# Turning the q and k tiles of an attention and mixture-of-experts kernel as F32R instead of F32 operands

## What is computed

```python
def _attn_ref(q, k, v, centroids):            # q, k, v: (2, 8, 768, 64); centroids: (8, 16, 64)
    q_assign = argmax(einsum('bhsd,hcd->bhsc', normed(q), normed(centroids)), axis=-1)
    k_assign = argmax(einsum('bhsd,hcd->bhsc', normed(k), normed(centroids)), axis=-1)
    mask = q_assign[:, :, :, None] == k_assign[:, :, None, :]
    scores = where(mask, q @ k.T / 8, -1e9)
    return softmax(scores) @ v

x = attention output, as 1536 tokens of 512
idx = argmax(normed(x) @ normed(expert_emb).T / tau)      # one of 8 experts for each token
x = gate * (relu(x @ w1[idx]) @ w2[idx])                  # w1: 512 to 1024, w2: 1024 to 512
out = ((x @ w_a) * (x @ w_b)) @ w_out                     # 512 to 1536 and back
```

## Time and profile before

| | us |
|---|---|
| median of three executions | 971.63 |
| lowest, highest | 966.73, 979.37 |
| the profiled execution | 973.64 |
| span of its instructions | 971.8 |
| mean granted TensorE clock, of full speed | 0.939 |

### The profile page before, as it was taken

The page is one execution under the profiler, slowest core; times in us unless marked ns, Lnnn a source line. Parts: engine busy times, 40 slices in busy tenths (PEclk is TensorE's granted clock), DMA queues, the critical chain, the costliest instruction groups (busy, mean ns, idle before and its releaser), DMA issues.

```text
span 971.8 us, 11830 instructions
## 1 busy us (share of the span) xinstructions
PE 880.1 (91%) x4205; PEld 620.6 (64%) x4206; DVE 513.0 (53%) x683; ACT 293.4 (30%) x558; POOL 225.8 (23%) x175
## 2 busy tenths in 40 slices
PE   5799989999899989509999999969999999999998
PEld 2455555555445554207777777757888888888886
DVE  4667888777888755626566665534321311131111
ACT  3133333333333334503434444423121211121111
POOL 6045655655665442150000000020000100000000
PEclk9579999988999989858999999988999999999999
DMA  4122222222221121366555555652000200010001
GB/s 123 50 70 67 71 68 75 73 78 72 75 67 48 48 82 60 140 222 237 199 199 204 202 196 206 211 183 74 0 1 1 87 1 1 0 44 1 1 1 43
DMA packets 41105, 86.93 MB, mean 89 GB/s; under 512 B 4216, under 2 KB 10584, under 8 KB 41056
## 3 DMA queue, kind: packets, MB, share of 16 engines
q1 hardware_dynamic: 39136, 79.99, 25.4%
q0 software_dynamic: 1920, 6.29, 1.9%
HBM read 60.53 MB, written 17.83 MB: 81 GB/s over the span
## 4 chain that ended last, share of the span: by engine, by line
PE 80%; DVE 11%; issue 6%; DMA 1%; ACT 0%; SPq 0%; DVEq 0%; POOL 0%; ACTq 0%
PE bank L1414 7%; PE bank L1415 7%; PE bank L1416 7%; PE bank L1214 4%; PE pair L1161 4%; PE bank L1354 3%; PE first_pair L1345 3%; PE first_pair L1346 3%; PE first_pair L1347 3%; PE bank L1355 3%; PE bank L1356 3%; PE first_pair L1199 3%; PE first_pair L1201 3%; DVE has_tmp L890 2%; PE bank L1131 2%
## 5 line engine op out<-in xcount | busy, mean ns | idle before, releaser
L1088 DVE TENSOR_TENSOR g_sb<-bank,a_sb 128x512 f32<-128x512 f32 x36 | 24.9, 692 | 196.7 <-PE bank L1416 196.7
L1414 PE MATMUL bank<-x_hi,wt 128*128 128x512 f32 x288 | 115.0, 399 | 1.4 <-DVE x_lo L1057 1.4
L1415 PE MATMUL bank<-x_lo,wt 128*128 128x512 f32 x288 | 114.6, 398 | 0.0
L1416 PE MATMUL bank<-x_hi,wt 128*128 128x512 f32 x288 | 114.5, 398 | 0.0
L844 DVE TENSOR_REDUCE neg_max<-pair 128x1 f32<-128x768 f32 x93 | 88.5, 951 | 45.8 <-PE pair L1161 45.7
L346 POOL TENSOR_TENSOR prob_sum<-prob_sum,prob 128x768 f32<-128x768 f32 x56 | 102.5, 1831 | 11.6 <-ACT prob L582 9.6
L959 DVE TENSOR_TENSOR wt<-w_raw,wt 128x2048 fp32r<-128x2048 f32 x41 | 92.9, 2287 | 10.2 <-ACT wt L661 9.8
L582 ACT ACTIVATE prob<-first_pair 128x384 f32<-128x384 f32 x128 | 59.6, 486 | 83.7 <-PE first_pair L1201 56.6
L1214 PE MATMUL bank<-prob,v_sb 128*64 128x384 f32 x384 | 83.8, 520 | 0.0
L1161 PE MATMUL pair<-kc,qb 96*128 96x384 f32 x186 | 61.7, 417 | 6.1 <-DVE neg_max L844 5.2
L1414 PEld LDWEIGHTS bank<-x_hi,wt 128*128 128x128 f32 x288 | 54.6, 190 | 15.1 <-DVE x_lo L1057 1.8
(11 more groups left out here) (212 smaller groups left out, 1666.1 us busy)
## 6 DMA issues: line engine op xcount, KB each, us to landing
w_raw<-in_moe_w_dram SPq DMA_DIRECT2D x32, 1024.0 KB, 5.2
x_slots<-zeros SPq DMA_DIRECT2D x10, 512.0 KB, 3.7
x_slot<-x_slots SPq DMA_DIRECT2D x18, 256.0 KB, 4.0
y_slots<-y_sb SPq DMA_DIRECT2D x16, 256.0 KB, 4.5
q_raw<-in_q_dram SPq DMA_DIRECT2D x16, 192.0 KB, 2.4
k_raw<-in_k_dram SPq DMA_DIRECT2D x16, 192.0 KB, 2.5
v_sb<-in_v_dram SPq DMA_DIRECT2D x16, 192.0 KB, 2.3
qb<-qa SPq DMA_DIRECT2D x16, 192.0 KB, 2.6
```

The lines of the kernel that those rows point to most:

```text
L1414: pe.matmul(to[:, :], w[0], x2_hi[:, kk, :], start=(kk == 0), stop=False)
L1415: pe.matmul(to[:, :], w[0], x2_lo[:, kk, :], start=False, stop=False)
L1416: last = pe.matmul(to[:, :], w[1], x2_hi[:, kk, :], start=False, stop=(kk == KD - 1))
```

## The change

A second identity, `ident_r`, is declared as F32R. DVE writes it in the setup with one more copy (128 by 128), placed between L786 and L787, and raises a new semaphore `setup_ident`. PE waits for that at the head of its program, behind its wait for `setup_in`. The transposes of L1131 take the tile as F32R, as it is declared, with `ident_r` as moving operand, and write through an F32R view of the bank; ACT and DVE read the bank as F32 as before. Pool's two subtractions (L496, L500) write to the F32R tile without the view as F32, so their results are rounded to F32R. The other transposes keep F32 and `ident`.

```diff
+        ident_r = sb("ident_r", [P, P], F32R)
...
+        setup_ident = sem("setup_ident")
...
             def low_parts(n):
...
-                pool.tensor_tensor(q_split[s][:, :, D:2 * D].bitcast(F32),
+                pool.tensor_tensor(q_split[s][:, :, D:2 * D],
                                    q_raw[s][:].rearrange("p (t d) -> p t d", t=NT),
                                    q_split[s][:, :, 0:D].bitcast(F32), ALU.subtract).then_inc(lo_ready, 1)
...
-                pool.tensor_tensor(k_split[s][:, :, 0:D].bitcast(F32),
+                pool.tensor_tensor(k_split[s][:, :, 0:D],
...
             dve.tensor_copy(ident_bf[:], ident)
+            dve.tensor_copy(ident_r[:], ident).then_inc(setup_ident, 1)
             dve.tensor_copy(upper_bf[:], cst[:, C_UP:C_UP + P])
...
             pe.wait_ge(setup_in, 64)
+            pe.wait_ge(setup_ident, 1)
...
-                        last = pe.transpose(at[:, i * P:(i + 1) * P], src[:, t, :].bitcast(F32), ident)
+                        last = pe.transpose(at[:, i * P:(i + 1) * P].bitcast(F32R), src[:, t, :], ident_r[:])
```

## The result

The median after is 980.99 us (974.54 to 991.06, 20 executions), that before beside it on the same chips 970.96 (965.01 to 979.37, 20). The ratio is 1.0126 with an interval of 1.0105 to 1.0146: 1.3% slower, where 0.3% faster was forecast. The profiled execution took 981.93 us, its span is 980.1, the mean granted clock 0.925. Against the profiled execution before that is 8.3 us more.

A forecast was written before the change was run, and what follows sets the result against it. PE, 91% busy, was taken to bound the kernel, with DVE sharing the attention rounds' chain. Transposes -5.0, setup +0.3, Pool 0 and clock +1.9 gave -2.8: 969 us against the median; 957 to 982 held most cases.

The forecast's parts named there:

- What bounds a round: Attention round of 21.16 us: waits run through DVE, PE's two k units, then DVE; q units only border a pause.
- The clock: Pause before L1181: one more round at half clock for a while, +1.9 us; ends -7.8 and +11.7.
- The second rival: Attention rounds: the longer pause makes the clock fall in all ten rounds, +7.0 us, 979; chance 0.15.
- The transposes: L1131: F32R step 0.070 us instead of 0.109, 5.9 us gained on the chain of waits, 5.0 let through.
- the cut from 5.9 to 5.0: Transpose gain on the chain reduced for passage through DVE's row maxima and cast, Pool's delays and ACT's copies.
- Rival (1): L1131: F32R transposes keep the F32 step of 0.109 us, leaving only setup's +0.3, 972; chance 0.22.
- Rival (3): L1131: the longer F32R weight load does not overlap, +7.1 us, with the setup 979; chance 0.08.
- Rival (4): Pool's subtractions: rounding to F32R costs threefold, +20 us over 13 rounds, 987; chance 0.04.
- Rival (5): Attention rounds: the clock falls in no round, -12.5 us in all, 959; chance 0.11.
- The setup: Kernel start: PE waits for DVE's identity copy of 0.6 us and begins near 8.7; +0.3 us, ends 0 and 1.0.
- What was to be seen: Expected profile signs, among them a pause before L1181 near 1.6 us and five of ten rounds with a fallen clock.
- A difference behind 400 us: Sign that the forecast is wrong: time differing late in the kernel, where nothing is changed.

The follow-up runs named there:

- only-q: The changed kernel with the k transposes (units 2 and 3) back in F32, only q turned as F32R: 988.77 us, ratio 1.0225 to the kernel before.
- only-k: The changed kernel with the q transposes (units 0 and 1) back in F32, only k turned as F32R: 975.88 us, ratio 1.0097 to the kernel before.

## Why the prediction was wrong, point by point

The forecast was 969 us, 0.3% faster; measured were 981. The sum was -5.0 + 0.3 + 0 + 1.9 = -2.8, and the profiled difference is +8.3.

**What bounds a round** held. The chain goes through DVE, the two k units and DVE again; q's units are off it. The only-q and only-k runs show just that: 21.14 and 21.07 us a round at full clock.

**The clock, the step that failed.** "I count one more fallen round, +1.9" was five more, from four to nine of ten, and the cost of the falls went from 7.8 to 17.4 us: +9.6 instead of +1.9. The text had the mechanism (less PE work, a longer pause, the fall right behind it), and put the right end on it (+11.7), but took one round of the six because equal rounds had fallen and not fallen. That spread was the sign: a round which falls or does not with the same work stands at the edge, and then a small shortening takes nearly all of them over it. The second rival, +7.0 and 979, is what happened, and it had a chance of 0.15. The filled pause shows that the clock is the cause of the loss, and the left-out transposes that less PE work is enough for it; the forecast should have been that rival's. That its 979 is so near to 981 is in part luck: its -5.0 was too large, and 2.1 us of the profiled difference lie behind the router's first product. Nor was four of ten a firm count to start from: the kernels with all transposes in F32 show three, four and seven in one execution each. The pause grew by 0.13 us (1.34 to 1.47), not by 0.2 to 0.3.

**The transposes, the term that was mis-sized.** The step was nearly right: 0.06 to 0.08 us against the 0.070 that was forecast, and the record 226 ns against "near 0.22". What did not come is the passage to the round. It was to be 20.8 to 21.0 us at full clock and is 21.09: 0.12 us a unit were to be gained, 0.24 a round, and 0.07 were. In the first k unit of the timelines the third transpose started 0.27 us behind the first before and 0.20 after, but the next product started 0.03 us behind the third one before, and 0.09 after. So of 0.07 us only 0.02 reached that product. In the second unit the third transpose starts 0.09 us sooner, and 0.06 of it reach the second L1199 behind it (L1203 after); of the two units together 0.08 us reached the work behind them. With the clock held, the whole is 0.08 us a round. At half clock 0.15 and 0.17 us a unit were passed on, of the 0.27 forecast. With 0.04 at full clock and 0.16 at half, the forecast's own sum would be 16 x 0.04 + 15 x 0.16 = 3.0 us, an estimate, where it had 5.9 and let 5.0 through. The reason that was given for the cut from 5.9 to 5.0, delays on DVE, Pool and ACT, is not where it was lost; it was lost on PE itself, at the end of each unit.

**Rival (1)**, no faster transpose, is out by the steps of 0.06 to 0.08. **Rival (3)**, a longer load, is out: the load stays at 138 ns. **Rival (4)**, Pool, is out: 1.00 and 1.01 us, as the forecast had it at nothing. **Rival (5)**, no falls, came only with the filler, which gave 960.

**The setup** held: PE began at 9.33 us instead of the 8.7 forecast, since the copy began at 8.20 and took 1.03 us and not 0.6. L1115 (before L1111) started at 15.94, between the 15.7 and 16.7 that were named and 0.26 later than before, where 0.3 was forecast; PE had stood idle for 2.01 us before it, which hid the rest. The setup alone is 1.0009 (0.9963 to 1.0054).

**What was to be seen** in the profile after: the pause of "near 1.6 us" is 1.47; five of ten fallen rounds are nine. A difference behind 400 us was named as a sign of being wrong, and 2.1 of the 8.3 us lie behind the router's first product, from the same clock.

**Open** is why q's change alone lets every round fall, where q's and k's together leave one free; the equal distances of 23.9 us are only observed. Left open too is whether the slower router stretch is more than this one execution's. And no run shows what filler in the pauses before the rounds would bring, where the clock stood at half from 26 to 53 us even in the changed kernel with ten transposes in each round's pause.

## What to carry to other kernels

Before work is taken off an engine that already waits, look at the granted clock of equal stretches one by one: where some have fallen behind a pause and others have not, the kernel stands at an edge, and less work of TensorE in the round can cost more than it saves. Count them in more than one execution: kernels with the same transposes had three, four and seven of ten. Price such a term by the case in which all of them fall, and split a change into the part on the chain (k here, 0.07 us shorter a round) and the part beside it (q here, next to nothing to gain). A pause of TensorE that recurs every round can be filled with transposes that nobody reads; here ten of them in the pause made the kernel before 1.1% faster (959.45 us), and the same ten just behind it made it 2.4% slower.

## What the runs showed of the hardware that was not expected

- Transposes hold the granted clock where they fill a pause, and they raise it by themselves: it went from 0.50 to 1.00 at 409.9 us, with nothing but transposes on PE since 407.1. With ten in the pause all rounds from 53 to 370 us were at 1.00; with the same ten behind it, and with four fewer a round, all fell.
- Falls often recur at one distance. In the only-q kernel and in the one with filler behind the pause they begin 23.9 us apart, eight and more times in a row, and in the changed kernel four times. In the kernel with filler behind the pause all ten rounds take on that length, 23.84 to 23.90 us, in the only-q kernel four, 23.88 to 23.90. Both were slower than their neighbours, 988.77 and 992.6 us.
- An F32R transpose follows the one before it sooner than an F32 one does (0.06 to 0.08 against 0.109 us for a tile of 128), with the same shortest weight load of 138 ns, and an F32R result costs Pool nothing (1.00 to 1.01 us). But the product behind the first k unit starts later after the unit's last transpose (0.09 us instead of 0.03), so that in this kernel 0.07 us a round remained of it at full clock.
